# Turn tables made by GpSimd, last weight pieces split a chunk sooner, and a row of its own for the second tile

## What is computed

```python
# 1. linear attention with decay, B, H, S, D = 4, 8, 768, 48
for t in range(S):
    cur = einsum('bhd,bhe->bhde', u[None] * k[:, :, t], v[:, :, t])
    y[:, :, t] = einsum('bhd,bhde->bhe', r[:, :, t], state + cur)
    state = w[None, :, :, None] * state + einsum('bhd,bhe->bhde', k[:, :, t], v[:, :, t])
x = y.transpose(0, 2, 1, 3).reshape(3072, 384)
# 2. mixture of 8 experts, one expert for each token, hidden width 1024
logits = x @ w_gate; expert_idx = argmax(logits, axis=1)
for e in range(8):
    out[expert_idx == e] = gate_w * (maximum(xe @ w1[e], 0.0) @ w2[e])
# 3. feed-forward with ELU, hidden width 2048
h = x @ w_in; g = where(h > 0, h, exp(minimum(h, 0)) - 1); return g @ w_out
```

## Time and profile before

| what | before |
|---|---|
| median of 3 runs | 893.48 us (890.81 to 893.85) |
| profiled execution, its own time | 888.82 us |
| span of its trace | 887.1 us |
| mean granted TensorE clock | 0.992 |
| PE busy | 851.8 us, 96% of the span |
| PEld / DVE / POOL / ACT busy | 770.8 / 411.5 / 399.2 / 246.4 us |
| chain that ended last, shares | PE 78%, issue 12%, DVE 4%, POOL 3%, DMA 2% |

### The profile page before, as it was taken

How to read it: one execution, slowest core, us unless ns; L and a number is a source line. 1 busy time by engine, 2 the same in 40 slices (tenths; PEclk the granted TensorE clock), 3 DMA queues, 4 the chain that set the end, 5 groups by cost and what they waited for, 6 DMA issues and landing times.

```text
span 887.1 us, 16841 instructions
## 1 busy us (share of the span) xinstructions
PE 851.8 (96%) x5278; PEld 770.8 (87%) x5278; DVE 411.5 (46%) x842; ACT 246.4 (28%) x514; POOL 399.2 (45%) x286
## 2 busy tenths in 40 slices
PE   5999989879999999999999999999999999999996
PEld 5888988669999999999988899988999989998895
DVE  7888997625444444434335553332333232332221
ACT  3333232212222222222223343222332223232221
POOL 7677677207575734437102223423423422433424
PEclk9999999989999999999999999999999999999998
DMA  7877986353445335164121000100100100000000
GB/s 181 235 230 235 238 237 192 126 178 117 149 145 177 118 117 176 48 228 147 37 63 45 19 19 10 45 19 1 54 18 1 44 27 0 35 0 0 36 1 36
DMA packets 48991, 83.96 MB, mean 95 GB/s; under 512 B 6816, under 2 KB 27040, under 8 KB 48544
## 3 DMA queue, kind: packets, MB, share of 16 engines
q1 hardware_dynamic: 35808, 60.59, 22.8%
q10 hardware_dynamic: 10048, 13.04, 4.6%
q0 software_dynamic: 3072, 9.46, 2.8%
HBM read 65.92 MB, written 17.15 MB: 94 GB/s over the span
## 4 chain that ended last, share of the span: by engine, by line
PE 78%; issue 12%; DVE 4%; POOL 3%; DMA 2%; SPq 1%; POOLq 0%; ACT 0%; ACTq 0%; DVEq 0%
PE bank L1462 10%; PE bank L1464 10%; PE bank L1463 9%; PE bank L1574 6%; PE bank L1576 6%; PE bank L1575 6%; PE bank L1593 5%; PE bank L1595 5%; PE bank L1594 5%; PE bank L1487 3%; PE bank L1393 2%; PE bank L1348 2%; PE bank L1382 2%; PE bank L1407 2%; POOL glo L669 2%
## 5 line engine op out<-in xcount | busy, mean ns | idle before, releaser
L669 POOL TENSOR_TENSOR glo<-gf,ghi 128x512 fp32r<-128x512 f32 x96 | 123.8, 1290 | 303.9 <-ACT ghi L1291 303.9
L1072 DVE TENSOR_SCALAR he<-he 128x512 f32<-128x512 f32 x96 | 41.0, 427 | 241.0 <-ACT he L1309 240.9
L1309 ACT ACTIVATE he<-bank 128x512 f32<-128x512 f32 x96 | 57.5, 599 | 253.5 <-PE bank L1576 253.5
L1593 PE MATMUL bank<-wout_hi,ghi 128*128 128x384 f32 x376 | 126.1, 335 | 0.3 <-issue 0.3
L1595 PE MATMUL bank<-wout_hi,glo 128*128 128x384 f32 x376 | 126.1, 335 | 0.0
L1594 PE MATMUL bank<-wout_lo,ghi 128*128 128x384 f32 x376 | 126.0, 335 | 0.0
L1574 PE MATMUL bank<-x2hi,win_hi 128*128 128x512 f32 x288 | 115.7, 402 | 0.0
L1576 PE MATMUL bank<-x2hi,win_lo 128*128 128x512 f32 x288 | 114.1, 396 | 0.0
L1575 PE MATMUL bank<-x2lo,win_hi 128*128 128x512 f32 x288 | 113.5, 394 | 0.0
L1462 PE MATMUL bank<-w_sb,hThi 128*128 x248 | 87.5, 353 | 4.8 <-DVE hTlo L938 2.9
L1464 PE MATMUL bank<-w_sb,hTlo 128*128 x248 | 84.6, 341 | 0.0
(11 more groups left out here) (214 smaller groups left out, 1502.5 us busy)
## 6 DMA issues: line engine op xcount, KB each, us to landing
w_raw_up<-w SPq DMA_DIRECT2D x12, 768.0 KB, 6.2
w_raw_down<-w SPq DMA_DIRECT2D x12, 768.0 KB, 7.0
w_raw<-w SPq DMA_DIRECT2D x24, 256.0 KB, 4.1
y_rows<-ye ACTq DMA_DIRECT2D x31, 192.5 KB, 2.5
xg<-x_sorted ACTq DMA_DIRECT2D x30, 193.0 KB, 2.8
k_in<-kT SPq DMA_DIRECT2D x48, 96.0 KB, 3.4
r_in<-rT SPq DMA_DIRECT2D x48, 96.0 KB, 3.7
kn_in<-kn SPq DMA_DIRECT2D x24, 192.0 KB, 3.8
```

The lines of the kernel that those rows point to most:

```text
L669: pool.tensor_tensor(glo[f % GS][:, :], gf[f % 2][:, :], ghi[f % GS][:, :].bitcast(F32), ALU.subtract).then_inc(s.g_lo, 1)
L1309: act.activation(he[f % 2][:, :], bank[1 + f % 2][:, :], ACT.Exp).then_inc(s.exp_done, 1)
L1593: pe.matmul(to, ghi[f % GS][:, rows], wout_hi[:, f, :], start=(f == 0), stop=False)
```

## The change

- **Turn tables.** `turns_a` to `turns_e` leave DVE. POOL makes the same tables and three more values in a new function `turn_tables`, called in chunk 13 behind its products and ahead of its scatter: 29 instructions, of 8 columns or one, but for two of 64, with six waits of POOL on its own results (`plink`). `turns_ok` is now signalled by POOL.
- **Weight pieces.** From chunk 14 on, ACT and POOL take piece n - 1 in chunk n, with pieces 12 and 13 both in chunk 14, and pieces 22 and 23 both in chunk 23. Nothing is left behind the loop. The order of SP's loads is as before.
- **Early tile.** `gate_and_id(0)` and `v_hT(0)` on DVE move from behind `tile_row` to ahead of `past`.
- **Own row for the second tile.** DVE makes `next_row` with four small instructions right behind `fill_row`; ACT loads tile 1 with it, without waiting for `rows_ok`.
- **Fills.** SP reads the experts of all turns into registers ahead of its wait for `fill_rows_ok`, so that each `fill` reads one register. Turn 3 has a signal of its own, and ACT loads tile 3 after it, behind `a_x(1)` and ahead of `a_relu(1)`; the wait for the other fills stands ahead of the loop over the tiles.

```diff
--- before
+++ after
-            return [n] if n < FIRST else ([n - 2] if n >= FIRST + 2 else [])
+            if n < FIRST:
+                return [n]
+            if n < FIRST + 2:
+                return []
+            return {FIRST + 2: [n - 2, n - 1], NT - 1: [n - 1, n]}.get(n, [n - 1])
...
@@ -449,16 +463,15 @@
                 if n == FIRST + 2:
                     sp.wait_ge(s.first_ok, 1)
                     expert = sp.value_load(first_expert[0:1, 0:1], min_val=0, max_val=E - 1)
-                    raw_piece(FIRST, expert)
-                if n < FIRST:
-                    raw_piece(n, None)
-                elif n >= FIRST + 2:
-                    raw_piece(n - 1, expert)
-            raw_piece(NT - 1, expert)
+                for m in split_now(n):
+                    raw_piece(m, expert)
+            sp.wait_ge(s.turns_ok, 1)
+            turns = [sp.value_load(turn_expert[0:1, turn:turn + 1], min_val=0, max_val=E - 1) for turn in range(E)]
             def fill(turn, done):
-                e = sp.value_load(turn_expert[0:1, turn:turn + 1], min_val=0, max_val=E - 1)
+                e = turns[turn]
                 row = sp.value_load(fill_row[0:1, bass.ds(e, 1)], min_val=0, max_val=(E + 1) * REG - P)
                 sp.dma_start(x_sorted[bass.ds(row, P), :], zeros[:, :]).then_inc(done, 16)
...
-            sp.wait_ge(s.turns_ok, 1)
             sp.wait_ge(s.fill_rows_ok, 1)
             for turn in range(2):
                 fill(turn, s.fill_in)
             for c in range(XT):
                 sp.wait_ge(s.x_out[c], 16 * B // 2)
             fill(2, s.fill2_in)
-            for turn in range(3, E):
+            fill(3, s.fill3_in)
+            for turn in range(4, E):
                 fill(turn, s.fills_in)
             load_raw(2, True)
...
                         products(n + 1, (NC // 2) * b + (c + 1) // 2, (c + 1) % 2, fresh and c == 0)
                     for m in split_now(n):
                         first_experts(m)
+                    if n == FIRST + 1:
...
+            def turn_tables():
+                pool.wait_ge(s.first_ok, 1)
+                pool.tensor_scalar(pull[:, :], most[:, :], float(P), None, ALU.is_lt)
+                pool.tensor_scalar(is_first[:, :], iota_e[:, :], first[:, 0:1], None, ALU.is_equal)
+                pool.tensor_scalar(to_first[:, :], iota_e[:, :], 1.0, first[:, 0:1], ALU.add, ALU.is_equal)
+                pool.tensor_scalar(first_base[:, :], first[:, :], -float(REG), float(E * REG), ALU.mult, ALU.add)
+                pool.tensor_scalar(first_1[:, :], first[:, :], 1.0, None, ALU.add)
+                plink(pool.tensor_scalar(from_first[:, :], iota_e[:, :], first[:, 0:1], None, ALU.is_ge))
+                pool.tensor_scalar(self_first[:, :], is_first[:, :], first[:, 0:1], None, ALU.mult)
+                pool.tensor_scalar(pull_first[:, :], is_first[:, :], pull[:, 0:1], None, ALU.mult)
+                pool.tensor_scalar(self_1[:, :], is_first[:, :], first_1[:, 0:1], None, ALU.mult)
+                pool.tensor_scalar(first_mul[:, :], first[:, :], pull[:, 0:1], None, ALU.mult)
+                pool.tensor_scalar(other_row[:, :], first_base[:, :], float(-E * REG), None, ALU.add)
+                plink(pool.tensor_copy(first_slot[:, :], pull[:, :]))
+                pool.tensor_tensor(from_first[:, :], from_first[:, :], self_first[:, :], ALU.add)
+                pool.tensor_tensor(gap[:, :], self_1[:, :], to_first[:, :], ALU.subtract)
+                pool.tensor_tensor(first_mul[:, :], first_mul[:, :], first[:, :], ALU.subtract)
+                plink(pool.tensor_tensor(other_row[:, :], other_row[:, :], pull[:, :], ALU.mult))
+                pool.tensor_tensor(turn_of[:, :], iota_e[:, :], from_first[:, :], ALU.subtract)
+                pool.tensor_scalar(gap[:, :], gap[:, :], -float(REG), float(REG), ALU.mult, ALU.add)
+                pool.tensor_scalar(first_tile_row[:, :], first_mul[:, :], float(REG), float(E * REG), ALU.mult, ALU.add)
+                pool.tensor_scalar(other_row[:, :], other_row[:, :], float(E * REG), None, ALU.add)
+                plink(pool.tensor_scalar(to_first[:, :], iota_e[:, :], first[:, 0:1], None, ALU.is_le))
+                pool.tensor_tensor(ahead[:, :, :], turn_of[:, :].unsqueeze(1).to_broadcast([P, E, E]),
+                                   turn_of[:, :].unsqueeze(2).to_broadcast([P, E, E]), ALU.subtract)
+                pool.tensor_tensor(row_step[:, :], first_base[:, :], other_row[:, :], ALU.subtract)
+                plink(pool.tensor_tensor(self_1[:, :], iota_e[:, :], to_first[:, :], ALU.subtract))
+                pool.tensor_scalar(first_mul[:, :], pull[:, :], -float(P), float(P), ALU.mult, ALU.add)
+                pool.tensor_scalar(ahead[:, :, :], ahead[:, :, :], 0.0, None, ALU.is_lt)
+                plink(pool.tensor_copy(self_1[:, 0:1], first[:, :]))
+                pool.tensor_copy(turn_expert[:, :], self_1[:, :])
+                pool.tensor_tensor(row_step[:, :], row_step[:, :], first_mul[:, :], ALU.add).then_inc(s.turns_ok, 1)
...
@@ -625,8 +682,6 @@
                 batch(b, b == 0, b == B - 1)
                 if b == 0:
                     routing_tables()
-            for m in (NT - 2, NT - 1):
-                first_experts(m)
             for c in range(LAST, NC):
                 scatter_x(B - 1, c, B)
...
-            def turns_a():
-
-                dve.tensor_scalar(pull[:, :], most[:, :], float(P), None, ALU.is_lt)
...
-            def turns_e():
-
-                tlink(dve.scalar_tensor_tensor(rev_best[:, :], first[:, :], pull[:, 0:1], first[:, :], ALU.mult, ALU.subtract))
...
                         pick_first()
-                    if FIRST < n <= FIRST + 5:
-                        (turns_a, turns_b, turns_c, turns_d, turns_e)[n - FIRST - 1]()
...
@@ -968,8 +986,13 @@
             place(LAST, NC - LAST, B, B - 1, True)
             dve.wait_ge(s.full_ok, 2)
+            dve.wait_ge(s.turns_ok, 1)
             rlink(dve.tensor_copy(n_e[:, :], counts))
             dve.tensor_tensor(fill_row[:, :], n_e[:, :], first_row[:, :], ALU.add).then_inc(s.fill_rows_ok, 1)
+            rlink(dve.tensor_tensor(from_first[:, :], n_e[:, :], is_first[:, :], ALU.mult))
+            rlink(dve.tensor_reduce(n_first[:, :], from_first[:, :], AX.X, ALU.add))
+            rlink(dve.tensor_scalar(n_first[:, :], n_first[:, :], float(P), row_step[:, 0:1], ALU.is_gt, ALU.mult))
+            dve.tensor_scalar(next_row[:, :], n_first[:, :], other_row[:, 0:1], None, ALU.add).then_inc(s.next_row_ok, 1)
             rlink(dve.tensor_tensor(more[:, :, :], n_e[:, :].unsqueeze(2).to_broadcast([P, E, NT]),
                                     full_at[:, :, :], ALU.is_gt))
             rlink(dve.tensor_reduce(tiles_e[:, :], more[:, :, :], AX.X, ALU.add))
@@ -981,15 +1004,14 @@
             rlink(dve.tensor_tensor(end_e[:, :], start_e[:, :], tiles_e[:, :], ALU.add))
             dve.scalar_tensor_tensor(jump_e[:, :], tiles_e[:, :], float(P), gap[:, :], ALU.mult, ALU.add)
             rlink(dve.tensor_copy(index[:, 0:1], pulled_at[:, :]))
+            gate_and_id(0, 0, True)
+            v_hT(0, 0, True)
             rlink(dve.tensor_tensor(past[:, :, :], index[:, :].unsqueeze(2).to_broadcast([P, NI, E]),
                                     end_e[:, :].unsqueeze(1).to_broadcast([P, NI, E]), ALU.is_ge))
             rlink(dve.tensor_tensor(skip[:, :, :], past[:, :, :], jump_e[:, :].unsqueeze(1).to_broadcast([P, NI, E]), ALU.mult))
             rlink(dve.tensor_reduce(skipped[:, :], skip[:, :, :], AX.X, ALU.add))
             rlink(dve.scalar_tensor_tensor(skipped[:, :], index[:, :], float(P), skipped[:, :], ALU.mult, ALU.subtract))
             dve.tensor_scalar(tile_row[:, :], skipped[:, :], first_base[:, 0:1], float(REG), ALU.add, ALU.max).then_inc(s.rows_ok, 1)
-            gate_and_id(0, 0, True)
-            v_hT(0, 0, True)
...
             exps(LAST, NC - LAST, B, B - 1)
-            for m in (NT - 2, NT - 1):
-                expert_highs(m)
...
+            def load_x(i, slot, at=None):
+                row = act.value_load(tile_row[0:1, bass.ds(i, 1)] if at is None else at[0:1, 0:1], min_val=0, max_val=(E + 1) * REG - P)
                 act.dma_start(xg[slot][:, :], x_sorted[bass.ds(row, P), :]).then_inc(s.xg_in[slot], 16)
...
             a_hT(0, 0, True)
             for c in range(XT):
                 act.wait_ge(s.x_out[c], 16 * B // 2)
+            act.wait_ge(s.next_row_ok, 1)
+            act.wait_ge(s.fill_in, 32)
+            load_x(1, 1, next_row)
             act.wait_ge(s.rows_ok, 1)
-            act.wait_ge(s.fill_in, 32)
-            load_x(1, 1)
             act.wait_ge(s.fill2_in, 16)
             next_x(2, 0)
             a_x(1, xhi[1], True)
+            act.wait_ge(s.fill3_in, 16)
+            next_x(3, 1)
             a_relu(1, 1, True)
             a_x(2, xhi[0], False)
             a_hT(1, 1, True)
-            act.wait_ge(s.fills_in, 16 * (E - 3))
-            next_x(3, 1)
```

(26 more changed lines are left out.)

21 lines of the change are left out of this document (removed).

## The result

The changed kernel takes 885.16 us, median of 5 runs (883.79 to 887.06), beside 892.83 us (888.98 to 893.85, 5 runs) for the kernel before: a ratio of 0.9928, 95% interval 0.9909 to 0.9947. By the ratio that is 6.4 us of 893; the two medians lie 7.7 us apart. Both are more than the 0.5% that can be told apart. The time is inside the forecast's range and 0.7 us above its median, but the saving falls short of the 9.0 us of the sum. The profiled execution has a span of 883.5 us, against 887.1.

A forecast was written before the change was run, and what follows sets the result against it. PE hardly ever waits; three places were to gain: attention, a late h, a late tile, pauses also lowering its clock. Gains 1.3 + 1.15 + 6.5 = 9.0 us from 888.82 give 879.8; median set at 884.5 us, range 880.5 to 890.0.

The forecast's parts named there:

- Fills and tile 3: Between tiles 1 and 3: quicker fills and an earlier load of tile 3 remove idle time and slow clock, 6.5 us.
- the worst case of the text: For tile 3: it lands only with the four raw DMAs. For attention: tables of 7.0 us, net -1.9 us.
- Rival 2: Tile 3 stays late behind raw weights that go out first; gain only 2.5 us, 891.0 us; chance 0.07.
- Early h: Early tile: DVE takes up h ahead of the tables, so first_down starts 1.15 us sooner; possible clock gain not counted.
- Pieces sooner: Weight pieces a chunk sooner: nothing in attention, as chunks 8 to 11 ran so; 0.8 us for DVE's queue, off the path.
- Turn tables: Attention, chunks 14 to 18: 2.1 us gained by leaving DVE, 0.8 us lost through POOL, net 1.3 us.
- The text's slack of 3.0 us: Chunk 13's tables: POOL's 0.8 us of idle plus 2.2 us before SP takes up its load absorb part of the block.
- a third of it reaches PE: Attention: SP's queue comes 2.5 us late behind POOL's tables, and PE is assumed to lose a third, 0.8 us.
- the text's own signs of being wrong: POOL's block over 7 us; PE waiting in chunks 15 to 17 for ACT's row copy or a load; L1457 waiting for xg.
- Rival 3: POOL's tables in attention: a first call adds about 6 us, tables 11.5 us; chance 0.13 together with Rival 2.
- Rival 4: Chunk 15 waits in POOL's queue because small arithmetic is dear; 0.6 us an instruction gives about 898 us; chance 0.04.
- Rival 1: Queues hide the tables in attention and pauses vanish to the ceiling: 12.9 us gained, 880.6 us; chance 0.17.

The follow-up runs named there:

- e2: Kernel before with only the fills' registers read ahead, a signal for turn 3's fill, and the early load of tile 3: 881.50 us, ratio 0.9928.
- e9: Changed kernel with tables split over chunks 13 and 22, but gate_and_id(0) and v_hT(0) back behind tile_row: 882.65 us, ratio 0.9902.
- e11: e6 run again, unaltered, in another group: 880.13 us, ratio 0.9883.
- e6: Changed kernel with five table instructions left on POOL in chunk 13 and the 24 others moved to chunk 22: 879.16 us, ratio 0.9894.
- e7: Kernel before with only the weight pieces taken a chunk sooner: 889.79 us, ratio 1.0003.
- e4: Changed kernel with POOL's 29 table instructions in six parts over chunks 13 to 18: 880.86 us, ratio 0.9928.
- e5: Changed kernel run again, unaltered, in another group: 882.74 us, ratio 0.9931.
- e8: Changed kernel with POOL's block of tables run twice in chunk 13: 889.18 us, ratio 1.0010.
- the split kernel: Changed kernel with five table instructions in chunk 13 and 24 in chunk 22, run as e6 (879.16 us) and e11 (880.13 us).
- e3: Changed kernel with the turn tables back on DVE in chunks 13 to 17, five extra operations added: 883.26 us, ratio 0.9954.
- e1: Kernel before with only the turn tables moved from DVE to POOL, one block in chunk 13: 891.05 us, ratio 1.0037.

## Why the prediction was right, and where it was not

**Direction, median and place of the gain were right; the attention term had the wrong sign.**

- *Fills and tile 3*, forecast 6.5 us: measured 6.9 us, 6.4 us by e2's ratio. Most steps came as the text has them, counted from the transposes of tile 0's h (162.02 before, 166.47 after): the load of tile 3 goes out at 10.3 us (text 10, before 17.5), fills follow each other by 1.15 us (text 1.1, before 1.87). The raw weights go out at 11.4 us, 3.6 us sooner than before and not 4.5 to 5.6; so they stand behind tile 3's load, and the worst case of the text, tile 3 landing only with them, did not arise. The load has landed at 180.0, 7 us ahead of its transposes at 187.32. Of the ceiling only the 1.1 us between 10.60 and 9.53 remains. Rival 2, tile 3 still late, did not occur.
- *Early h*, forecast 1.15 us: hTlo 1.10 us sooner behind hThi in the change, and 1.0 us from tile 0 to tile 1 (14.59 against 15.59); between 1.1 and 2.8 us by e9 beside e11 and e6. The clock behind it did fall, as the text had left open: matmuls of L1484 take 0.53 us each from 170.10 to 172.98 and 0.34 us from 173.50 on, and from 171 to 173 the clock is 0.50.
- *Pieces sooner*, forecast "nothing": right beside the change as a whole, but the reason given was wrong. That chunks 8 to 11 bear such a schedule says nothing of chunks 14 to 18, where DVE makes tables: alone (e7) the part takes 4.1 us more there (29.65 against 25.52). Its trace shows 1.6 us given back, from tile 0 to tile 2; why the runs of e7 are all the same level with the kernel before (1.0003) is open. Only the tables' leaving makes the part harmless in these chunks.
- *Turn tables*, forecast 2.1 - 0.8 = 1.3 us: this is the step that failed. Moving them away is worth 2.1 us, as e4 and e6 show (23.28 and 23.25 us). What the block costs on POOL was mis-sized twice. Its length is 7.3 us, outside the bounds of 3.4 to 7.0: the price of 8 columns was taken from an iota, 0.14 us, but an operation with a column of scalars takes 0.3 us and any other about 0.2, 0.25 us an instruction with its waits. The text's slack of 3.0 us held: 7.3 - 3.0 = 4.3 us, and SP issues the load of k 4.4 us late, at 100.84 instead of 96.47. (Two errors in it cancel: before, POOL had 1.8 us of idle ahead of its two products, not 0.8, and some 0.9 us more goes by between the chunk's old scatter at 89.22 and the block, and behind the block.) The second mistake is "a third of it reaches PE", 0.8 us, which the text took from no row. PE stands for v 3.3 us in the change (1.87 and 1.38) and 2.0 us in e5, and behind the first wait the clock is lower, which the term did not hold at all. Measured: 2.1 gained and 3.5 to 4.9 us paid in the four chunks (26.99 us in e5, 28.3 in the first), where the worst case of the text was 4.0. e8 shows that there is no slack left behind the first block. Two of the text's own signs of being wrong came true: a block over 7 us, and PE waiting for a load behind chunk 14.
- *The sum.* 9.0 us would have been about the gain of the change with its tables where they do no harm: the split kernel has 9.4 and 10.4 us by its two ratios. What it has over the change is 3.3 us in e5's group. By the stages the change gets 6.9 + 1.0 and loses 1.5 us in attention in e5 (26.99 against 25.52), 6.4 us, as the ratio says. That the median was met within 0.7 us is in part luck: the sum is 1.3 us over the 7.7 us of the medians, and the 893.48 us it starts from lie 0.65 us over the median beside the change.
- *Rival 3*, a first call that costs some 6 us by the rule of the Trainium skill (GPSIMD Engine Reference, Instruction dispatch): the first tensor_scalar of POOL takes 0.25 us and the second starts 0.23 us behind it. No run here shows such a price. *Rival 4* had the mechanism and the place right (attention waits in POOL's queue, and SP's loads behind it) at a price between forecast and rival: 0.25 us an instruction, not 0.4. Its stall, block less 3.0 us, fits too: 4.3 us, measured 3.5 to 4.9.
- *Rival 1*, the queues hide the tables: no; PE's waits for v contradict it.

**Open:** what DVE waited for in the two unnamed waits (1.9 and 2.2 us, in two of thirteen profiled executions; not in the other copy of the change); the exact share of the pieces' schedule; and what the row of its own for the second tile is worth, which no run takes away alone.

## What to carry to other kernels

Work moved to an idle engine must be priced by what is queued behind it there, and that engine's share of busy time does not say it: POOL was busy under half of the span, yet in the stage of the tables it released SP's loads, and a second block of 7 us was paid in full. Cut such a block by due time: five instructions were wanted soon, 24 could wait nine chunks for a place where nothing stands behind them. Spreading it over six chunks was no cure. And look for waits for "all" and for a place in a queue that stand ahead of one urgent DMA: here they were worth as much as the whole change.

## What the runs showed of the hardware

- Small arithmetic on POOL in the change: 0.18 to 0.22 us for 1 or 8 columns, 0.29 to 0.33 us if a scalar comes from a column in SBUF (0.25 us for the first of all), 0.25 us from one to the next on average (29 in 7.3 us). DVE does the same in 0.14 to 0.23 us in e3, but for two instructions beside a busy POOL.
- An operation of 8 columns on DVE can last as long as POOL's neighbour: with two SBUF inputs 1.84 and 1.19 us in e7 and 1.33 in e3, and a cast with one input 0.87 us in e3, up to 113.03 where POOL's instruction ends at 113.01.
- A register read from SBUF on SP costs 0.72 us: with one read instead of two, the fills follow each other by 1.15 us instead of 1.87.
- Single pauses of PE within full work were often followed by a stretch at a lower clock, but their length alone does not say when. After 1.87 (change), 1.92 (e7), 2.04 (e5) and 2.13 us (e3) it came; in e1 it came after 1.40 us (0.50 from 122 to 124 us) and not after 1.71 us; after the 1.38 us in the change and 0.8 to 1.0 us in e4 it did not. Busy time of e7 behind its pause, mean clock 0.57:

```profile
105.00:113.00 8.00, 7.90 (x56) 7.32 (x57) 6.15 (x16) 2.07 (x6) 3.46 (x4) 0.57 0.81 228
```
